# FFN 2's hidden product as seven products of half size, with weights combined on the chip

## The reference

```python
x = attention(q, k, v, p)                 # 8 batches of 576 tokens, 8 heads of 64
xn = x / sqrt(mean(x * x) + 1e-6) * rms_g # FFN 1, 1536 hidden columns
x = (silu(xn @ w_gate) * (xn @ w_val)) @ w_out
h = x @ w_in                              # FFN 2, w_in 512 x 2048: the product that changes
return (h * cos(h)) @ w_out2              # w_out2 2048 x 512
```

## Time and profile before

| what | value |
|---|---|
| median of 3 runs | 1854.01 us (1852.22 to 1857.13) |
| span of the profiled execution | 1856.4 us |
| FFN 2 begins (first matmul) | 1064.82 us |
| FFN 2's matmuls | 3456 |
| DMA traffic in all | 131.81 MB, mean 71 GB/s |
| queue that carries nearly all of it | 131.09 MB, 19.5% of 16 engines |

### The profile page before, as it was taken

How to read it: one execution, slowest core, us unless ns; L and a number is a source line. 1 busy time by engine, 2 the same in 40 slices (tenths; PEclk the granted TensorE clock), 3 DMA queues, 4 the chain that set the end, 5 groups by cost and what they waited for, 6 DMA issues and landing times.

```text
span 1856.4 us, 25532 instructions
## 1 busy us (share of the span) xinstructions
PE 1831.5 (99%) x9306; PEld 1494.8 (81%) x9306; DVE 1012.2 (55%) x1556; ACT 668.5 (36%) x1081; POOL 482.0 (26%) x399
## 2 busy tenths in 40 slices
PE   8799999999999999999999999999999999999999
PEld 6677777777888888888888878888888888888887
DVE  3754564555454233322222376767767676767675
ACT  2345545544432221211111134343434343434343
POOL 3501111101344343311111632222222222222222
PEclk9999999999999999999999999999999999999999
DMA  6533324330322322211111310010101010101000
GB/s 222 167 128 148 147 73 150 121 122 23 127 98 79 125 97 96 85 68 62 46 50 59 122 57 23 24 46 0 45 0 45 0 45 0 45 0 45 0 23 23
DMA packets 40869, 131.81 MB, mean 71 GB/s; under 512 B 3696, under 2 KB 4720, under 8 KB 32880
## 3 DMA queue, kind: packets, MB, share of 16 engines
q1 hardware_dynamic: 40816, 131.09, 19.5%
HBM read 83.89 MB, written 47.19 MB: 71 GB/s over the span
## 4 chain that ended last, share of the span: by engine, by line
PE 96%; DVE 3%; ACT 1%; issue 0%; POOL 0%; DVEq 0%; ACTq 0%
PE ps L442 31%; PE ps L444 30%; PE ps L443 30%; PE ps L503 1%; PE ps L460 1%; PE ps L636 1%; PE ps L489 1%; PE ps L475 0%; PE ps L545 0%; PE ps L522 0%; ACT xt L745 0%; DVE xraw L1036 0%; DVE xlo L1041 0%; DVE tmp L1016 0%; DVE angle L1175 0%
## 5 line engine op out<-in xcount | busy, mean ns | idle before, releaser
L424 POOL TENSOR_TENSOR glo<-gate,ghi 128x512 fp32r<-128x512 f32 x144 | 191.7, 1331 | 588.5 <-ACT ghi L914 588.5
L395 POOL TENSOR_TENSOR hlo<-prod,hhi 128x512 fp32r<-128x512 f32 x108 | 147.0, 1361 | 700.7 <-ACT hhi L774 700.7
L1046 DVE TENSOR_TENSOR sig<-sig,ps 128x512 f32<-128x512 f32 x108 | 74.2, 687 | 370.9 <-ACT sig L769 370.9
L914 ACT ACTIVATE ghi<-gate 128x512 fp32r<-128x512 f32 x144 | 91.1, 632 | 405.2 <-DVE gate L1184 405.2
L442 PE MATMUL ps<-wout,ghi 128*128 128x512 f32 x576 | 224.8, 390 | 2.6 <-POOL glo L424 2.6
L442 PE MATMUL ps<-xhi,win 128*128 128x512 f32 x576 | 225.2, 391 | 0.0
L444 PE MATMUL ps<-xhi,win 128*128 128x512 f32 x576 | 224.4, 390 | 0.0
L443 PE MATMUL ps<-xlo,win 128*128 128x512 f32 x576 | 224.4, 390 | 0.0
L443 PE MATMUL ps<-wout,ghi 128*128 128x512 f32 x576 | 224.4, 390 | 0.0
L444 PE MATMUL ps<-wout,glo 128*128 128x512 f32 x576 | 224.4, 390 | 0.0
L1167 DVE TENSOR_SCALAR turns<-ps 128x512 f32<-128x512 f32 x144 | 99.4, 690 | 169.5 <-PE ps L444 168.4
(11 more groups left out here) (111 smaller groups left out, 3173.8 us busy)
## 6 DMA issues: line engine op xcount, KB each, us to landing
xraw<-x_scratch SPq DMA_DIRECT2D x17, 1024.0 KB, 5.3
k_sb<-k_t SPq DMA_DIRECT2D x16, 576.0 KB, 5.2
q_sb<-q_t SPq DMA_DIRECT2D x8, 1152.0 KB, 5.1
x_scratch<-xt SPq DMA_DIRECT2D x8, 1152.0 KB, 4.3
xn_scratch<-xraw SPq DMA_DIRECT2D x9, 1024.0 KB, 3.8
part_scratch<-tmp SPq DMA_DIRECT2D x9, 1024.0 KB, 5.1
xraw<-xn_scratch SPq DMA_DIRECT2D x9, 1024.0 KB, 6.8
tmp<-part_scratch SPq DMA_DIRECT2D x9, 1024.0 KB, 4.8
```

What stands on the lines that cost most here:

```text
L395: nc.gpsimd.tensor_tensor(hlo[f % RING1][:], prod[f % 2][:], hhi[f % RING1][:].bitcast(F32), ALU.subtract).then_inc(h_lo, 1)
L424: nc.gpsimd.tensor_tensor(glo[f % RING2][:], gate2[f % 2][:], ghi[f % RING2][:].bitcast(F32), ALU.subtract).then_inc(g_lo, 1)
L914: nc.scalar.activation(ghi[e % RING2][:], gate2[e % 2][:], ACT.Copy).then_inc(g_hi, 1)
L1046: nc.vector.tensor_tensor(sig[f % 2][:], sig[f % 2][:], ps[:, GATE_BANK, :], ALU.mult).then_inc(gv_free, 1)
```

## The change

FFN 2's hidden product works on quads: two chunks of hidden columns (A, B) at once, the 512 features as two halves, the 512 tokens as two halves. Of this 2 x 2 x 2 product, Strassen's form (in Winograd's variant) makes seven products, `P1` to `P7`, of 128 hidden columns, 256 features and 256 tokens each. A product is 2 slices x 3 = 6 matmuls of 256 columns. The second product, `output2`, keeps its shape.

- Combined weights. In half 2, tiles 0 to 3, SP loads the raw weights of each of 8 quads (`load_w2`), GpSimd makes the four combined pieces (`sum_w2`, 256 elements each), rounds all seven (`round_w2`, 1792 elements) and forms the remainders (`rest_of_w2`), and SP stores them to DRAM (`store_w2`, 1.835 MB a quad). The loading and splitting of `wout2` moves to tiles 4 to 7 and to the start of FFN 2. In FFN 2 SP streams each quad's weights back for every tile into two buffers, in three transfers (`win2_a`: P1, P3, P7; `win2_b`: P6, P2, P5; `win2_c`: P4).
- Tokens. GpSimd makes four combined pieces of the next tile's tokens in quads 3 to 6 (`sum_x`); ScalarE rounds seven pieces in quad 7 and quad 0 (`round_x2`), and GpSimd, no longer VectorE, forms the seven remainders (`rest_of_x2`).
- PSUM. P1 goes into half a bank (the base); ScalarE copies it out (`keep_base` 0), P6 is added and copied (1), P5 is added and copied (`shared`, 2). VectorE's `add_second` adds `shared` to P3 and P7, which gives chunk B's hidden values (`hid2`, in SBUF); P4 is issued in the next quad (`last_product`), and `add_first` gives chunk A's from P2, P4 and the kept bases.
- The chain of a unit (one chunk of a quad) reads `hid2` in SBUF. ScalarE multiplies by 1 / 2 pi (`turn`), VectorE rounds in one instruction and does the rest of `reduce_unit`, ScalarE Abs and Sin, VectorE the gate, ScalarE the rounding, GpSimd the remainder. A quad's two units pass through it while TensorE works on the next quad, and their outputs are issued two quads later.

```diff
+QUADS = FC2 // 2
+PRODUCTS = 7
+HT, HK = TT // 2, KC // 2
+P1, P3, P7, P6, P2, P5, P4 = range(PRODUCTS)
+UNITS = 4
+EARLY_WOUT2 = 12
...
+            def quad2(t, q):
+                i = t * QUADS + q
+                more = not is_last(t) or q < QUADS - 2
+                if more:
+                    sp.wait_ge(second_filled, i + 1)
+                    load_win2(q + 2, P1, P6, win2_a)
+                if not (is_first(t) and q == 0):
+                    sp.wait_ge(quad_filled, i)
+                    load_win2(q + 1, P4, P4 + 1, win2_c)
+                if more:
+                    sp.wait_ge(base_filled, 3 * i + 3)
+                    load_win2(q + 2, P6, P4, win2_b)
+                if q == 1 and not is_last(t):
+                    sp.wait_ge(xc_lo, t * PRODUCTS + PRODUCTS)
                     sp.wait_ge(x2_stored, 16 * TILES)
                     sp.dma_start(xraw[:], x2_dram[t + 1]).then_inc(x_loaded, 16)
+                if q == 2 and not is_first(t):
+                    store_out(t - 1)
...
+            def sum_w2(n):
+                raw = w2_raw[n % 2]
+                pool.wait_ge(w2_loaded[n % 2], 48 * (n // 2 + 1))
+                for to, plus, minus in ((P5, PRODUCTS, P1), (P7, P3, PRODUCTS), (P6, P3, P5), (P4, P2, P6)):
+                    if to == P6:
+                        pool.wait_ge(w2_sums, 4 * n + 1)
+                    elif to == P4:
+                        pool.wait_ge(w2_sums, 4 * n + 3)
+                    nc.gpsimd.tensor_tensor(raw[:, to], raw[:, plus], raw[:, minus], ALU.subtract).then_inc(w2_sums, 1)
+            def round_w2(n):
+                pool.wait_ge(w2_sums, 4 * n + 4)
+                wait_used(pool, w2_stored, 16 * (n - 1))
+                nc.gpsimd.tensor_scalar(w2_out[n % 2][:, :, 0], w2_raw[n % 2][:, 0:PRODUCTS], 1.0, 0.0, ALU.mult,
+                                        ALU.add).then_inc(w2_hi, 1)
+            def rest_of_w2(n):
+                pool.wait_ge(w2_hi, n + 1)
+                out_n = w2_out[n % 2]
+                nc.gpsimd.tensor_tensor(out_n[:, :, 1], w2_raw[n % 2][:, 0:PRODUCTS], out_n[:, :, 0].bitcast(F32),
+                                        ALU.subtract).then_inc(w2_combined, 1)
...
+                    if u < QUADS // 2 and f < 4:
+                        n = 2 * u + f // 2
+                        if f % 2 == 0:
+                            sum_w2(n)
+                            round_w2(n)
+                        else:
+                            rest_of_w2(n)
+                    if QUADS // 2 <= u < TILES - 1 and f < 3:
+                        if u == QUADS // 2 and f == 0:
+                            pool.wait_ge(w2_stored, 16 * QUADS)
+                        split_weights(W2_FIRST + 3 * (u - QUADS // 2) + f)
+                    if is_last(u) and f == 2:
+                        for j in range(4):
+                            sum_x(0, j)
...
+            def quad2(t, q):
+                n = 2 * (t * QUADS + q) - 2
+                some = not (is_first(t) and q == 0)
+                if q == QUADS - 1 and not is_last(t):
+                    for j in (P1, P3, P7):
+                        rest_of_x2(t + 1, j)
+                if some:
+                    rest_of_gate(n, 2 * q % UNITS - 2)
+                if q == QUADS - 1 and not is_last(t):
+                    rest_of_x2(t + 1, P6)
+                if q == 0 and not is_first(t):
+                    rest_of_x2(t, P2)
+                    rest_of_x2(t, P5)
+                if some:
+                    rest_of_gate(n + 1, 2 * q % UNITS - 1)
+                if q == 0 and not is_first(t):
+                    rest_of_x2(t, P4)
+                if 3 <= q < QUADS - 1 and not is_last(t):
+                    sum_x(t + 1, q - 3)
+                if is_first(t) and q < 2:
+                    for i in range(2):
+                        split_late(EARLY_WOUT2 + 2 * q + i)
...
+            def multiply2(t, q, j, dst, first):
+                if q == 0:
+                    pe.wait_ge(xc_lo, t * PRODUCTS + j + 1)
+                i, w = q % 2, win2[q % 2]
+                for k in range(HK):
+                    mm = product(dst, w[:, j, 0, k, :], w[:, j, 1, k, :], xchi[j][:, k, :], xclo[j][:, k, :],
+                                 first and k == 0, k == HK - 1, onto=not first)
+                return mm
...
+            def last_product(t, q):
+                i = t * QUADS + q
+                pe.wait_ge(win2_c[q % 2], 16 * (t * (QUADS // 2) + q // 2 + 1))
+                pe.wait_ge(h_added, 2 * i + 1)
+                multiply2(t, q, P4, second_half(q, 1), False).then_inc(quad_filled, 1)
...
+            def quad2(t, q):
+                i = t * QUADS + q
+                back = None if is_first(t) and q < 2 else (t, q - 2) if q >= 2 else (t - 1, q + QUADS - 2)
+                before = None if is_first(t) and q < 1 else (t, q - 1) if q >= 1 else (t - 1, QUADS - 1)
+                loads = 16 * (t * (QUADS // 2) + q // 2 + 1)
+                if is_first(t) and q == 0:
+                    pe.wait_ge(gv_free, 2 * TILES * 2 * FH)
+                else:
+                    pe.wait_ge(base_kept, 3 * i)
+                pe.wait_ge(win2_a[q % 2], loads)
+                multiply2(t, q, P1, base_half(), True).then_inc(base_filled, 1)
+                multiply2(t, q, P3, second_half(q, 0), True)
+                multiply2(t, q, P7, second_half(q, 1), False).then_inc(second_filled, 1)
+                if before is not None:
+                    last_product(*before)
+                if back is not None:
+                    output2(*back, range(0, 3))
+                pe.wait_ge(win2_b[q % 2], loads)
+                pe.wait_ge(base_kept, 3 * i + 1)
+                multiply2(t, q, P6, base_half(), False).then_inc(base_filled, 1)
+                if back is not None:
+                    output2(*back, range(3, 6))
+                if before is not None:
+                    pe.wait_ge(h_added, 2 * i)
+                multiply2(t, q, P2, ps_halves[:, 2 * H11_BANK, :], True)
+                pe.wait_ge(base_kept, 3 * i + 2)
+                multiply2(t, q, P5, base_half(), False).then_inc(base_filled, 1)
+                if back is not None:
+                    output2(*back, range(6, 8))
+            quads(pe, quad2)
+            last_product(TILES - 1, QUADS - 1)
+            output2(TILES - 1, QUADS - 2, range(8))
+            output2(TILES - 1, QUADS - 1, range(8))
...
+            def keep_base(t, q, k):
+                i = t * QUADS + q
+                act.wait_ge(base_filled, 3 * i + k + 1)
+                dst = base[q % 2][:, k, :] if k < 2 else shared[q % 2][:]
+                nc.scalar.activation(dst, ps_halves[:, 2 * BASE_BANK, :], ACT.Copy).then_inc(base_kept, 1)
...
+            def turn(n, slot):
+                act.wait_ge(h_added, n + 1)
+                wait_used(act, g_lo, n - UNITS + 1)
+                nc.scalar.activation(angle[slot][:], hid2[slot][:], ACT.Copy, scale=INV_2PI).then_inc(turned, 1)
+            def cosine(n, slot):
+                act.wait_ge(reduced, 4 * n + 4)
+                nc.scalar.activation(angle[slot][:], angle[slot][:], ACT.Abs).then_inc(trig, 1)
+                act.wait_ge(trig, 2 * n + 1)
+                nc.scalar.activation(angle[slot][:], angle[slot][:], ACT.Sin, scale=-1.0, bias=half_pi[:]).then_inc(trig, 1)
...
+            def quad2(t, q):
+                n = 2 * (t * QUADS + q) - 2
+                slot = (2 * q - 2) % UNITS
+                before = None if is_first(t) and q < 1 else (t, q - 1) if q >= 1 else (t - 1, QUADS - 1)
+                more = q == QUADS - 1 and not is_last(t)
+                if q == 2 and not is_first(t):
+                    keep_out(t - 1, 2)
+                    keep_out(t - 1, 3)
+                if before is not None:
+                    turn(n, slot)
+                keep_base(t, q, 0)
+                if more:
+                    round_x2(t + 1, P1)
+                if before is not None:
+                    cosine(n, slot)
+                if more:
+                    act.wait_ge(second_filled, t * QUADS + QUADS)
+                    round_x2(t + 1, P3)
+                    round_x2(t + 1, P7)
+                if before is not None:
+                    turn(n + 1, slot + 1)
+                    round_gate(*before, 0)
+                if q == 0 and not is_first(t):
+                    act.wait_ge(quad_filled, t * QUADS)
+                    round_x2(t, P4)
+                keep_base(t, q, 1)
+                if more:
+                    round_x2(t + 1, P6)
+                if before is not None:
+                    cosine(n + 1, slot + 1)
+                keep_base(t, q, 2)
+                if more:
+                    round_x2(t + 1, P2)
+                    round_x2(t + 1, P5)
+                if before is not None:
+                    round_gate(*before, 1)
+                if q == 1 and not is_first(t):
+                    keep_out(t - 1, 0)
```

(61 more changed lines are left out.)

348 lines of the change are left out of this document (191 added, 157 removed).

## The result

The changed kernel takes 2031.7 us (median of 4 runs, 2030.7 to 2034.3) against 1854.2 (4 runs, 1852.2 to 1857.1): 1.096 times as long, 95% interval 1.094 to 1.097. The profiled execution's span is 2032.5 us.

What follows compares the result with a forecast made beforehand. TensorE's issue was taken to bound FFN 2 before, the VectorE-ScalarE loop with GpSimd's collisions after. 1064.8 + 958.8 + 2.5 = 2026.1 us span, less 2.4 gives 2024 us, 9% slower; range 1930 to 2090.

Steps and rivals of the forecast that it cites:

- TensorE's part: FFN 2: matmuls of 256 columns cost 0.120 us; 28.7 us saved over 72 quads, leaving 755.1 us of TensorE work.
- The work before FFN 2: Half 2: GpSimd makes the combined weights, 12 us in two chunks of 16.3 us, hidden behind TensorE, cost nothing.
- The loop and the collisions: FFN 2: VectorE-ScalarE loop of 10.25 us a quad, lengthened by GpSimd holding VectorE; 106.4 us a tile, 2024 us, chance 0.80.
- the timetable: Four engines' programs carried forward instruction by instruction with row durations; FFN 2 958.8 us.
- TensorE's waits: In FFN 2, about 200 us, put down to keep_base(2) before P1 and the remainder of x before P2 of quad 0.
- The rule that who comes second waits, less 0.15 us: VectorE and GpSimd on SBUF: the later one waits, less 0.15 us start-up; full blocking instead gives 2078 us.
- FFN 2's own start: Start of FFN 2: expected unchanged at 1064.8 us, the weights made before it making nothing late.
- VectorE's rounding in the earlier trace: Given as a VectorE operation with both sources in SBUF that GpSimd stretches, 1.13 us in place of 0.43.
- the clock in full: TensorE in FFN 2: clock granted in full as long as single waits stay near 1 to 2 us.
- (a): Rival, FFN 2: contention doesn't reach the loop; 88.2 us a tile, 1863 us, slower by 0.5%; chance 0.08.
- (b): Rival, FFN 2: TensorE stays the bound in every quad; 755.1 + 9 us, 1829 us, faster; chance 0.07.
- (c): Rival: worse than 2085 us, the stream or its waits on SP hold TensorE, or a loop wait was missed; chance 0.05.

Runs made afterwards that it cites:

- e3: The changed kernel with GpSimd's FFN 2 operations (gates' remainders from tile 1 on, token sums and remainders) on 64 of 512 columns: 1862.8 us.
- e5: The changed kernel without the two scalar_tensor_tensor of every unit in FFN 2, GpSimd as it was: 1861.9 us.
- e7: The changed kernel with the same instructions, but GpSimd's released by waits to where VectorE is idle in the loop: 1917.5 us.
- e1: The changed kernel with the gates' remainders moved from GpSimd to VectorE, into times when VectorE waits for Abs and Sin: 1929.1 us.
- e6: The changed kernel with add_second put ahead of the second gate on VectorE: 2096.9 us.
- e4: The changed kernel with ScalarE's wait for x2's last store moved from FFN 2's start to the first copy of the output: 2023.9 us.
- e9: Like e8, but P2's token remainder also on VectorE, and ScalarE's four output copies together in quad 2 behind the first turn: 1839.1 us.
- e2: The changed kernel with every transfer of combined weights in FFN 2 cut to one block of 128 columns, all waits kept: 2032.7 us.
- e8: e7 with e4's edit and five of the seven token remainders on VectorE, P6 and P2 staying on GpSimd: 1895.1 us.

## Why the prediction was right

**TensorE's part.** Eighteen matmuls of 256 columns from 1502.63 to 1504.67 start 0.120 us apart, as worked out from the 288 and 512 columns. TensorE's work starts FFN 2 at 1064.6.

**The work before FFN 2.** The sizes were off by little and the conclusion held. GpSimd in half 2 of the changed kernel (count, busy us, mean ns):

```profile
L512 POOL TENSOR_TENSOR w_out<-w_raw,w_out 128x1792 fp32r<-128x1792 f32 x8 | 32.4, 4050 | 0.0
L501 POOL TENSOR_TENSOR w_raw<-w_raw 128x256 f32<-128x256 f32 x32 | 22.9, 737 | 4.6 <-DMA w_raw<-w_in 4.0
...
L506 POOL TENSOR_SCALAR w_out<-w_raw 128x1792 fp32r<-128x1792 f32 x8 | 13.6, 1698 | 0.7
```

```profile
570.00:1064.00 494.00, 494.00 (x2181) 409.18 (x2180) 142.29 (x201) 101.65 (x173) 187.06 (x150) 1.00 0.32 119
```

4.05, 0.74 and 1.70 us against 4.5, 0.67 and 2.2; TensorE is busy for 494.00 of 494 us, so all of it is hidden.

**The loop and the collisions.** A tile is 106.2 us against 106.4, its quads within 0.8 us of the timetable's (quad 0: 14.0 against 14.8; the others within 0.4). VectorE's two `scalar_tensor_tensor` have means of 1.02 and 1.18 us where 1.0 and 1.2 were forecast, rounding and clamp 0.68 and 0.59 for 0.65 and 0.6. TensorE's waits were to be 200 us: the four lines above are 138, and the time in which it issues nothing is 967.9 - 2.5 - 755.1 = 210. The rule that who comes second waits, less 0.15 us, held for VectorE's 1.66: from 1560.63, GpSimd ends at 1560.35 + 1.39 = 1561.74, and 1561.74 + 0.69 - 0.15 = 1562.28 against 1562.29. By the Trainium skill (SBUF — State Buffer, Who interferes with whom) the second engine blocks fully; this trace agrees but for those 0.15 us, with which the forecast was nearer (2031.7 measured, 2024 against 2078). e3 and e5 show that both the collisions and the chain are needed, e7 that the place of GpSimd's work in time decides and not its amount, e1 that VectorE's own amount of work isn't the limit. e6, forecast within 0.4%, bears out the order of the loop through gate, its rounding and `turn`.

**What the steps had wrong.** The term that failed is FFN 2's own start: "FFN 2 should begin at 1064.8 as now" holds for TensorE, but ScalarE's program of FFN 2 begins with a wait for the last store of x2, so the first copy of the base came at 1071.89. The timetable had no such wait. e4 gives it as 7.8 us in the medians, as much as lies between forecast and result (7.7). That the two are so near is luck. In e4's profiled execution, with the wait gone, FFN 2 takes 1064.5 to 2021.1 less 2.5, which is 954.1 us, and the timetable had 958.8: elsewhere it was some 5 us too long. And the forecast took 2.4 us off its span, as the profiled span of the kernel before lies above the median. That profiled execution was a slow one: in later executions of the same kernel the time lies 2.0 us above the span of the same execution, and in those of the changed kernel 1.8.

The prediction says that VectorE's rounding in the earlier trace rows has both sources in SBUF. It has one source; that it stands still all the same is what the rows show, and the forecast for rounding and clamp rests on it.

The prediction expected the clock in full as long as single waits stay near 1 to 2 us. That did not hold. In quad 7 of every tile but the last TensorE waits 2.5 to 4.1 us for `shared`, and the clock is low behind it; but in three of these eight, the one shown above among them, it fell to half ahead of that wait, here at 1589. TensorE's last waits before were 1.5 us (until 1577.29) and 1.8 us (until 1587.78):

```profile
1586.00:1588.00 2.00, 0.22 (x1) 0.22 (x2) 1.10 (x3) 2.00 (x5) 2.00 (x2) 1.00 0.00 0
1588.00:1590.00 2.00, 2.00 (x10) 1.68 (x10) 1.97 (x2) 0.25 (x1) 2.00 (x2) 0.73 0.19 28
1590.00:1592.00 2.00, 1.07 (x3) 0.33 (x1) 1.97 (x2) 0.00 (x0) 2.00 (x2) 0.50 0.87 283
```

The mean is 0.96 in FFN 2. In this kernel it cost little: from quad 6's copy of `shared` to quad 7's are 16.7 to 16.8 us in every tile, whether the clock fell before the wait or in it, and the timetable, which has the full clock throughout, gave 16.8. The waits came from where they were expected, `shared` above all.

**The rivals.** (a) fell: its time is that of e3, where the contention is nearly gone. The match to the microsecond is in part luck, since e3 has ScalarE's late start, which (a) has not, and has the remainders of x early. (b) fell as stated, for the collisions hit the loop. Its sum for a kernel without them was 1829, with 9 us of start and end; e9 is at 1839, with 16. (c) fell: e2 shows the stream free.

## What to carry to other kernels

When TensorE is the bound, fewer and shorter matmuls pay only if the chain of the other engines for one turn of the loop stays below the new, shorter turn; add it up with its queue order before the edit (here 10.25 against 10.49 us, a margin smaller than the smallest collision in a quad, 0.5 us). Lay GpSimd's elementwise work, by waits on VectorE's progress, where VectorE is waiting anyway, and keep out of a paced queue what TensorE needs soon. And look at a matmul's price as a pitch and a fixed part: seven products for eight took 28.7 us off TensorE's 783.8 in FFN 2, and not the 49 (an eighth of its first half) that the count of columns gives.

## What of the hardware was not expected

- After TensorE had stood still for 4.1 us the granted clock was 0.50 for some 6 us after it went on, although it was busy throughout (1245.88 to 1251.8 in e8). Short gaps are no safeguard: in the changed kernel the clock fell to 0.50 at 1589 behind gaps of 1.5 and 1.8 us.
- GpSimd's `tensor_tensor` of 256 elements takes 0.74 us, not half of the 1.29 for 512; one of 1792 takes 4.05. The three lie near 0.19 us and 2.15 ns an element, an estimate from them.
- VectorE's `tensor_scalar` on fp32, with a single source in SBUF, is held up by GpSimd as the ones with two are (1.02 us for 0.43 at 1553.48); so was the rounding in the earlier trace rows.
